# A fourth expert's slot products are moved ahead of the tile loop, and the weight loads are reordered for them

## The chip, the cores and the metric

The kernel runs on one core of one Trainium2 chip. The metric is the device time of one execution in microseconds (us), smaller is better. TensorE is called PE, VectorE DVE, ScalarE ACT, GpSimd POOL and SyncE SP. SP issues all the large loads, and POOL issues the indirect gathers and scatter-adds.

## What is computed

Attention over 8 heads with a local band and a few global columns, then two mixture-of-experts layers on the same 1536 tokens of width 512. The first is a soft one (every token is written as a mixture of 32 slots, four for each of 8 experts), the second sends each token to its two best experts.

```python
x = attention(q, k, v)                       # 1536 x 512
logits = x @ phi                             # 32 slots
slot_input = softmax(logits, axis=0).T @ x
slot_out[e] = relu(slot_input[e] @ w1[e]) @ w2[e]        # 8 experts, 4 slots each
x = softmax(logits, axis=1) @ slot_out       # layer 1's output: c @ slot_out

top2, weights = two best experts of noisy(x @ w_gate, x @ w_noise)
for e in range(8):                           # layer 2: tokens routed to expert e
    h = relu(x[mask] @ w1[e])                # 512 -> 1024
    out[mask] += weight * (h @ w2[e])        # 1024 -> 512
```

## The kernel before, in words

The first layer's output is never written out. Since x is c (1536 by 32) times the 32 slot rows s, the product x @ w1[e] of the second layer is c @ (s @ w1[e]). The 32-row product s @ w1[e] is called here the slot products of expert e. `slots_up(e)` makes them on PE (line 1509 of the kernel before, 16 matmuls, which the trace lists as 32) in PSUM bank 6, and `store_g(e)` on ACT copies them to `g_rows`. For e above 0, `slots_up(e)` waits until `store_g(e - 1)` is done, because there is one bank.

Tokens are sorted by expert into tiles of 128; here there are 28 tiles. For each tile POOL gathers 128 rows of c by an indirect DMA, ACT or POOL spreads them four times into `c4`, PE transposes them (`transpose_c4`, line 1261), DVE copies the result to `c4T`, PE forms the hidden values (`hidden`, line 1563), ACT applies relu and rounds (`hidden_high`, line 866), DVE keeps the remainder (`hidden_low`, line 1213), PE multiplies with w2 in split precision (`down`, lines 1574 and 1577, once for each half), ACT scales the sum (`store_y`, line 885) and POOL adds it to the output by an indirect DMA (line 705). The w2 weights of an expert must first be split: ACT writes the high part (`split_high`, line 733), DVE the low part (`split_low`, line 1127).

The weights of layer 2 pass through a ring of four buffers of 2 MB. Unit numbers are: `up1` and `down1` are the w1 and w2 of the second expert (expert 1), `up2` and `down2` of expert 2, `up3` and `down3` of expert 3, and so on. `up3` takes the buffer of `up1`, and can be loaded once the products of expert 1 are made. Units after the first few are loaded in two DMAs of 1 MB, of which the second is issued when the first has landed (`load_unit`, line 464); `down1` and `up2` are loaded in one DMA of 2 MB. SP issues the loads in the order of a written list (`order`, line 504), and waits for `c4_ready` (the first gather has arrived and been spread) before one of them.

Every engine has its program written by hand in one order, and waits on semaphores in that order. Before the tile loop PE makes the products of experts 0, 1 and 2, the routing tables, then for tile 0 the transpose and the hidden values, and then the transpose for tile 1. Inside the loop, `slots_up(e + 1)` stands ahead of the first tile's `down` of expert e for the later experts (`starts`, with `UP_EARLY` as the first such expert).

Of the kernel before, what the change touches and what calls it, by code (L numbers as in the profile page):

```python
# [16 lines left out]
def attention_two_moe_layers(nc, q, k, v, n_global, n_local, phi, a_w1, a_w2,  # L17
# [11 lines left out]
    E, _, F = a_w1.shape  # L29
# [18 lines left out]
    DC = DM // P  # L48
# [3 lines left out]
    FIRST = 4  # L52
    ROW = SLOTS + E
    ZEROED = 2 * 16
    UP_EARLY = 3
    DOWN_EARLY = 1
    AHEAD = 4
    REST = 4
# [2 lines left out]
    EARLY = 6  # L61
# [10 lines left out]
    with ExitStack() as ctx:  # L72
# [256 lines left out]
        g_ready, g_stored = sems("g_ready g_stored")  # L329
# [112 lines left out]
        def _(sp):  # L442
# [58 lines left out]


            down1, up2, down2, up3, down3, up4 = range(2 * E + RING2 - 1, 2 * E + RING2 + 5)
            order = [*range(EARLY, down1), up2, down1, up3, down2, *range(down3, 4 * E)]
            sums_before = {down3: 1, up4: 3}
            for n in order:
                m = before_unit(n)
                if n == EARLY + 2:

                    sp.wait_ge(heads_ready, UPB * B)  # L510
                if n == EARLY + DURING:

                    sp.wait_ge(part_ready, 1)
                if n == up3:

                    sp.wait_ge(c4_ready, 1)
                if n in sums_before:

                    sp.wait_ge(out_added, ZEROED + 16 * sums_before[n])
                if m is not None:  # L520

                    layer, which, e = units[m]
                    if (layer, which) == (1, 2):
                        sp.wait_ge(w_rest_stored, REST)
                        sp.wait_ge(w_lo_stored, FC * (e + 1) - REST)
                    else:
                        sp.wait_ge({(0, 1): hid_ready, (0, 2): soft_down_done, (1, 1): g_ready}[layer, which], e + 1)
                load_unit(n)
# [200 lines left out]
        def _(act):  # L729
# [42 lines left out]
            with nc.scalar.Else():  # L772
                for j in range(3):
                    store_qk(0, j, j, bank[FIRST_BANKS[j]])
                for u in range(UPB * B + 5):
                    p, i = divmod(u, QB)
                    if u < UPB * B:
                        off = P if i == 0 else 0
                        for h in range(2):
                            act.wait_ge(logits_ready, 2 * u + h + 1)  # L780
                            own = prob[u % 4][:, h, off:]
                            last = nc.scalar.activation(own, own, ACT.Exp, bias=neg_max[:, u % 2, h:h + 1], scale=-1.0,  # L782
                                                        accum_out=row_sum[:, u % 4, h:h + 1])
# [46 lines left out]
            def store_g(e):  # L830
                act.wait_ge(g_ready, e + 1)
                copy(g_rows[:, e, :], bank[6][:, 0:FR]).then_inc(g_stored, 1)
# [13 lines left out]
            for c in range(REST):  # L846
                split_low(c)
            store_g(1)

            def place_first(n):  # L850

# [18 lines left out]
            for half in range(2):  # L870
                hidden_high(half, 0, used=False)
            place_first(2)
            store_g(2)

            for n in range(FIRST):
                act.wait_ge(first_arrived[n], 16)
# [380 lines left out]
        def _(pe):  # L1257
# [21 lines left out]
            with pe.If(narrow == 0):  # L1279
                with pe.Fori(0, B) as b, pe.Fori(0, PAIRS // 2) as pp2:  # L1280
                    for s in range(2):
# [9 lines left out]
                        with pe.Fori(0, QB) as i:  # L1291
                            pe.wait_ge(all_q, UPB * b + 2 * QB * pp2 + i + (QB * s + 1))
                            for h in range(2):
                                n = 2 * UPB * b + 4 * QB * pp2 + 2 * i + (2 * QB * s + h + 1)
                                own = slice(h * HD, (h + 1) * HD)
                                for c in range(2):
                                    blocks = slice(c * QB // 2, (c + 1) * QB // 2)
                                    last = mm(bank[1 + c][:, 0:S // 2], q_block[own, :], kT[s][own, blocks, P:WIN],
                                              start=True, stop=True)
                                last.then_inc(all_scores, 1)  # L1300
                                pe.wait_ge(all_probs, n)
                                for c in range(QB):
                                    last = transpose(bank[4 + 2 * c // QB][:, (c % HALF) * P:(c % HALF + 1) * P],
                                                     prob_all[:, c * P:(c + 1) * P])
# [4 lines left out]
                                for c in range(QB):  # L1309
                                    last = mm(bank[6][own, 0:P], v_own[s][:, h, c, :], probT_all[:, c, :],  # L1310
                                              start=(c == 0), stop=(c == QB - 1))
                            last.then_inc(heads_ready, 1)
            with pe.Else():
# [53 lines left out]
                for u in range(UPB * B + 4):  # L1367
# [5 lines left out]
                    if 1 <= i <= 3 and p + 1 < NPAIR:  # L1373
                        n = 3 * (p + 1) + i - 1
# [25 lines left out]
            for c in range(DC):  # L1400
                for r in range(NG):
                    last = mm(bank[4][r * SLOTS:(r + 1) * SLOTS, 0:TG], phi_sb[:, c, :], xT[:, r * TPG:(r + 1) * TPG, c, :],
                              start=(c == 0), stop=(c == DC - 1))
# [7 lines left out]
            for t in range(TPG):  # L1411
                last = transpose(bank[5][:, t * P:(t + 1) * P], lT.rearrange("s (p t) -> s t p", t=TPG)[:, t, :])
# [9 lines left out]
            for t in range(TPG):  # L1422
                last = transpose(bank[6][:, t * P:(t + 1) * P], dT[:, t * P:(t + 1) * P])
# [6 lines left out]
            for t in range(TPG):  # L1430
                for r in range(NG):
                    last = mm(bank[0][r * SLOTS:(r + 1) * SLOTS, :], d_tok[:, (t * NG + r) * SLOTS:(t * NG + r + 1) * SLOTS],
                              x_sb[:, r * TPG + t, :], start=(t == 0), stop=(t == TPG - 1))
# [64 lines left out]
            last.then_inc(gate_log_ready, 1)  # L1498


            def slots_up(e):

                if e:

                    pe.wait_ge(g_stored, e)
                wait_unit(pe, (1, 1, e))
                for c in range(DC):
                    for r in range(NG):
                        last = mm(bank[6][r * SLOTS:(r + 1) * SLOTS, 0:FR], sT[:, c, :],  # L1509
                                  weights((1, 1, e))[:, c, r * FR:(r + 1) * FR], start=(c == 0), stop=(c == DC - 1))  # L1510
                last.then_inc(g_ready, 1)


            def split_rest(c):
# [31 lines left out]
            def transpose_c4(n, used=True):  # L1546
                pe.wait_ge(c4_ready, n + 1)
                if used:

                    pe.wait_ge(c4T_stored, n)  # L1550
                transpose(bank[7][:, 0:P], c4[:]).then_inc(c4T_ready, 1)
# [30 lines left out]
            pe.wait_ge(w_rest_stored, REST)  # L1582
            keep_warm(8)
            transpose_c4(0, used=False)
            pe.wait_ge(g_stored, 1)
            hidden(0, 0, used=False)
            transpose_c4(1)

            def period(i, e, first, last):
                up_ahead, _ = starts(e, first)  # L1590
# [48 lines left out]
```

## Time and profile before

| what | value |
|---|---|
| median of 3 runs (lowest, highest) | 393.13 us (390.88, 398.73) |
| the profiled execution's own time | 392.51 us |
| its span in the trace | 389.8 us |
| mean granted clock of PE | 0.971 of full |
| PE busy | 362.6 us, 93% |
| POOL, DVE, ACT busy | 213.3, 192.7, 170.4 us |

The span is what the trace covers; the execution's own time is 2.7 us longer. The attention takes the first third, layer 1 ends near 163 us, routing and tables last until about 187 us, and the 28 tiles fill the rest.

### The profile page before, as it was taken

How to read it: one execution, taken by the hardware profiler on the slowest of the kernel's cores; microseconds unless marked ns; L12 is line 12 of the kernel's file. 1: busy time of each engine (PE TensorE's matmuls, PEld its weight loads, DVE VectorE, ACT ScalarE, POOL GpSimd, SP SyncE). 2: the span in 40 equal slices, each digit the busy share in tenths (PEclk: the TensorE clock that was granted, in tenths of full speed). 3: DMA queues.
4: the chain of work that ended last, by engine and by line, in shares of the span. 5: the costliest groups of instructions: out<-in, count | busy, mean ns of one | idle time of the engine just before them, and what ended most of it. 6: DMA issues, size and time to landing. Idle time of an engine off the chain costs nothing.

```text
span 389.8 us, 8657 instructions
## 1 busy us (share of the span) xinstructions
PE 362.6 (93%) x2892; PEld 251.6 (65%) x2892; DVE 192.7 (49%) x639; ACT 170.4 (44%) x429; POOL 213.3 (55%) x422
## 2 busy tenths in 40 slices
PE   6899999999997999589799999999999999999990
PEld 5566666666564443256577777777777777777770
DVE  2699988888853011068172452623525426254210
ACT  2566777776541110043273453524525336253310
POOL 3568866667811040011446777747766576766741
PEclk9699999999999999889899999999999999999996
DMA  7987999999799999998577899876869762332432
GB/s 161 238 243 224 222 268 298 279 258 374 278 401 347 401 398 387 398 405 330 174 268 170 249 269 250 236 170 145 267 145 209 224 139 34 43 47 32 57 43 38
DMA packets 71976, 88.85 MB, mean 228 GB/s; under 512 B 41616, under 2 KB 42112, under 8 KB 71936
## 3 DMA queue, kind: packets, MB, share of 16 engines
q1 hardware_dynamic: 66448, 79.84, 62.7%
q0 software_dynamic: 5200, 8.49, 15.4%
q8 instruction: 23, 0.38, 0.4%
q14 instruction: 17, 0.14, 0.1%
q10 hardware_dynamic: 288, 0.00, 0.0%
HBM read 77.33 MB, written 10.99 MB: 227 GB/s over the span
## 4 chain that ended last, share of the span: by engine, by line
PE 59%; DVE 16%; issue 15%; DMA 8%; ACT 1%; DVEq 1%; POOL 0%; POOLq 0%; ACTq 0%
PE y_bank L1574 26%; PE y_bank L1577 13%; DMA weight_ring<-in_moe_w 6%; PE h_banks L1563 5%; DVE arena L1031 4%; DVE row_sum L1039 4%; PE bank L1509 3%; PE bank L1261 2%; PE y_bank L1478 2%; DVE row_inv L1053 2%; PE h_banks L1446 2%; PE h_banks L1261 1%; DVE arena L933 1%; DVE arena L1047 1%; DMA counts_i<-in_n_local 1%
## 5 line engine op out<-in xcount | busy, mean ns | idle before, releaser
L1213 DVE SCALAR_TENSOR_TENSOR hT_lo<-h_banks,hT_hi 128x512 fp32r<-128x512 f32 x56 | 38.5, 689 | 110.3 <-ACT hT_hi L866 104.8
L1574 PE MATMUL y_bank<-w_hi,hT_hi 128*128 128x512 f32 x224 | 91.6, 409 | 0.8 <-ACT hT_hi L866 0.8
L1574 PE MATMUL y_bank<-w_lo,hT_hi 128*128 128x512 f32 x224 | 88.2, 394 | 0.0
L866 ACT ACTIVATE hT_hi<-h_banks 128x512 fp32r<-128x512 f32 x56 | 33.4, 597 | 98.8 <-PE y_bank L1577 51.8
L610 POOL TENSOR_TENSOR arena<-arena,row_inv 128x512 f32<-128x512 f32 (+1 forms) x48 | 49.5, 1032 | 29.2 <-DVE row_inv L1053 27.1
L547 POOL TENSOR_TENSOR turn_mark<-turn_mark 128x1 f32<-128x1 f32 x135 | 41.4, 310 | 38.1 <-DMA out_rows<-arena,add_row 12.6
L1577 PE MATMUL y_bank<-w_hi,hT_lo 128*128 128x512 f32 x224 | 59.9, 389 | 0.0
L782 ACT ACTIVATE arena<-arena,neg_max 128x256 f32<-128x256 f32 (+1 forms) x96 | 46.3, 483 | 26.8 <-DVE neg_max L1031 25.8
L705 POOL DMA_INDIRECT out_rows<-arena,add_row x28 | 44.8, 1599 | 14.1 <-issue 13.0
L1574 PEld LDWEIGHTS y_bank<-w_hi,hT_hi 128*128 128x128 f32 x224 | 44.2, 197 | 11.2 <-issue 3.0
L1574 PEld LDWEIGHTS y_bank<-w_lo,hT_hi 128*128 128x128 f32 x224 | 42.8, 191 | 7.9
L1577 PEld LDWEIGHTS y_bank<-w_hi,hT_lo 128*128 128x128 f32 x224 | 42.1, 188 | 8.8
L1031 DVE CUSTOM_DVE_ANT_0 arena<-h_banks,arena 128x256 f32<-128x256 f32 (+1 forms) x96 | 34.4, 395 | 11.7 <-issue 11.4
L675 POOL DMA_INDIRECT c_fetched<-slot_rows,fetch_row x27 | 31.0, 1150 | 15.0 <-issue 14.9
L1127 DVE TENSOR_TENSOR w_lo<-weight_ring,w_hi 128x512 fp32r<-128x512 f32 x60 | 38.0, 692 | 0.0
L1330 PE MATMUL h_banks<-arena 64*128 64x256 f32 (+1 forms) x192 | 34.6, 425 | 1.8 <-DVE neg_max L1031 1.0
L733 ACT ACTIVATE w_hi<-weight_ring 128x512 fp32r<-128x512 f32 x64 | 34.8, 621 | 0.0
L1261 PE MATMUL y_bank<-ident,arena 128*128 128x128 f32 x190 | 32.2, 289 | 0.7 <-POOL arena L610 0.4
L1047 DVE COPY arena<-y_bank 128x512 f32<-128x512 f32 (+1 forms) x48 | 30.5, 635 | 1.5 <-PE y_bank L1261 1.5
L1261 PEld LDWEIGHTS y_bank<-ident,arena 128*128 128x128 f32 x190 | 20.1, 142 | 16.5 <-issue 11.1
L733 ACT ACTIVATE arena<-h_banks 128x512 f32<-128x512 f32 (+1 forms) x36 | 17.2, 496 | 15.8 <-PE h_banks L1261 8.2
L1330 PEld LDWEIGHTS h_banks<-arena 64*128 64x128 f32 x192 | 15.8, 191 | 10.7 <-issue 6.2
(196 smaller groups left out, 494.6 us busy)
## 6 DMA issues: line engine op xcount, KB each, us to landing
weight_ring<-in_moe_w SPq DMA_DIRECT2D x16, 2048.0 KB, 13.2
weight_ring<-in_moe_w SPq DMA_DIRECT2D x22, 1024.0 KB, 5.5
arena<-in_moe_w SPq DMA_DIRECT2D x5, 2048.0 KB, 12.1
arena<-in_q SPq DMA_DIRECT2D x16, 192.0 KB, 5.8
arena<-in_k SPq DMA_DIRECT2D x16, 192.0 KB, 5.4
arena<-in_v SPq DMA_DIRECT2D x8, 384.0 KB, 4.8
out_rows<-zero_row SPq DMA_DIRECT2D x2, 1536.0 KB, 10.4
out_rows<-arena,add_row POOLq DMA_INDIRECT x28
```

The lines of the kernel that those rows point to most:

```text
L547: g.tensor_tensor(turn_mark[:, turns[0]:turns[0] + 1], turn_mark[:, 0:1], turn_mark[:, 0:1], ALU.add)
L610: g.tensor_tensor(prob[u % 4][:, :, off:], prob[u % 4][:, :, off:], row_inv[:, u % 4, :].unsqueeze(2).to_broadcast([P, 2, WIN - off]), ALU ...
L705: pool.indirect_dma_start(out=out, out_offset=bass.IndirectOffsetOnAxis(ap=add_row[k][:, 0:1], axis=0), in_=y_sb[:, k], in_offset=None, bo ...
L733: return nc.scalar.activation(o, i, ACT.Copy)
L782: last = nc.scalar.activation(own, own, ACT.Exp, bias=neg_max[:, u % 2, h:h + 1], scale=-1.0, accum_out=row_sum[:, u % 4, h:h + 1])
L1031: vec.tensor_tensor_reduce(out=prob[u % 4][:, h, off:], in0=score_bank(u, h)[:, off:WIN], in1=bias8[:, 2 * pp + h, n0:n0 + nb], scale=-SCA ...
L1127: vec.tensor_tensor(w_lo[e % 2][:, c, :], weights((1, 2, e))[:, c, :], w_hi[e % 2][:, c, :], ALU.subtract).then_inc(w_lo_stored, 1)
L1213: vec.scalar_tensor_tensor(hidden_of(hT_lo, half), h_banks[half][:, :, 0:FR], 0.0, hidden_of(hT_hi, half), ALU.max, ALU.subtract).then_inc ...
L1261: return nc.tensor.transpose(o, i, ident[:])
L1330: last = mm(score_bank(u, h)[:, off:WIN], qT[s][own, i * P:(i + 1) * P], kT[s][own, i, off:], start=True, stop=True)
L1574: mm(y_of(i), hT_hi[:, n, :], w[e % 2][:, n, :], start=(n == 0 and w is w_hi), stop=False)
L1577: last = mm(y_of(i), hT_lo[:, n, :], w_hi[e % 2][:, n, :], start=False, stop=(n == FC - 1))
```

## The change

The slot products of expert 3 leave the tile loop. Their 16 matmuls are issued before it, in two halves: eight after the transpose for tile 0, and eight after the transpose for tile 1. ACT stores the products of expert 2 earlier (they must be out of the bank) and those of expert 3 where it stored those of expert 2. SP loads `up3` ahead of `down1`, and the wait for the first gather moves from `up3` to `down1`.

```diff
-    UP_EARLY = 3
+    UP_EARLY = 4
...
-            order = [*range(EARLY, down1), up2, down1, up3, down2, *range(down3, 4 * E)]
+            order = [*range(EARLY, down1), up2, up3, down1, down2, *range(down3, 4 * E)]
...
-                if n == up3:
+                if n == down1:
 
                     sp.wait_ge(c4_ready, 1)
...
             store_g(1)
+            store_g(2)
...
             place_first(2)
-            store_g(2)
+            store_g(3)
...
-            def slots_up(e):
-
-                if e:
+            def slots_up(e, chunks=range(DC)):
+
+                if e and 0 in chunks:
 
                     pe.wait_ge(g_stored, e)
                 wait_unit(pe, (1, 1, e))
-                for c in range(DC):
+                for c in chunks:
                     for r in range(NG):
                         last = mm(bank[6][r * SLOTS:(r + 1) * SLOTS, 0:FR], sT[:, c, :],
                                   weights((1, 1, e))[:, c, r * FR:(r + 1) * FR], start=(c == 0), stop=(c == DC - 1))
-                last.then_inc(g_ready, 1)
+                if DC - 1 in chunks:
+                    last.then_inc(g_ready, 1)
...
             transpose_c4(0, used=False)
+            slots_up(3, range(DC // 2))
             pe.wait_ge(g_stored, 1)
             hidden(0, 0, used=False)
             transpose_c4(1)
+            slots_up(3, range(DC // 2, DC))
```

PE before the tile loop, from the products of expert 2 to the first `down`, in the program before (bank is PSUM bank 6 for the products and bank 7 for the transposes, c holds the spread rows):

```order
L1509 MATMUL bank<-weight_ring,arena 32x256 x16
L1266 MATMUL h_banks<-ident 128x128 x8
L1261 MATMUL bank<-ident,c 128x128
L1563 MATMUL h_banks<-c4T,arena 128x128 x8
L1261 MATMUL bank<-ident,c 128x128
L1574 MATMUL y_bank<-w_hi_53,hT_hi 128x512
```

The same place in the changed program:

```order
L1510 MATMUL bank<-weight_ring,arena 32x256 x16
L1267 MATMUL h_banks<-ident 128x128 x8
L1262 MATMUL bank<-ident,c 128x128
L1510 MATMUL bank<-weight_ring,arena 32x256 x8
L1565 MATMUL h_banks<-c4T,arena 128x128 x8
L1262 MATMUL bank<-ident,c 128x128
L1510 MATMUL bank<-weight_ring,arena 32x256 x8
L1576 MATMUL y_bank<-w_hi_53,hT_hi 128x512
```

Eight matmuls of the products now stand ahead of the hidden values of tile 0, and eight ahead of its `down`.

SP's loads around the change, in the program before (in_moe2_w1 are up units, in_moe2_w2 down units; the first row is `up2`):

```order
L464 DMA weight_ring<-in_moe2_w1 128x4x1024 [waits g_ready]
L464 DMA weight_ring<-in_moe2_w2 128x8x512 [waits soft_down_done]
L464 DMA weight_ring<-in_moe2_w1 128x2x1024 [waits g_ready,c4_ready]
L464 DMA weight_ring<-in_moe2_w1 128x2x1024 [waits unit_loaded2]
L464 DMA weight_ring<-in_moe2_w2 128x4x512 [waits w_lo_stored,w_rest_stored]
```

And in the changed program:

```order
L464 DMA weight_ring<-in_moe2_w1 128x4x1024 [waits g_ready]
L464 DMA weight_ring<-in_moe2_w1 128x2x1024 [waits g_ready]
L464 DMA weight_ring<-in_moe2_w1 128x2x1024 [waits unit_loaded2]
L464 DMA weight_ring<-in_moe2_w2 128x8x512 [waits soft_down_done,c4_ready]
L464 DMA weight_ring<-in_moe2_w2 128x4x512 [waits w_lo_stored,w_rest_stored]
```

The two halves of `up3` now wait for no gather, and the 2 MB of `down1` do.

## Rows read from the trace of the kernel before

**Rows 1.** The page: busy time of PE, share of the span, instructions.

```profile
PE 362.6 (93%) x2892; PEld 251.6 (65%) x2892; DVE 192.7 (49%) x639; ACT 170.4 (44%) x429; POOL 213.3 (55%) x422
```

**Rows 2.** Chain of waits, tile loop: start us, us, what.

```profile
229.74 1.81 PE y_bank L1574 x8
...
232.46 0.66 PE h_banks L1563 x16
233.11 0.26 PE bank L1261
...
236.12 1.86 PE bank L1509 x32
237.99 2.04 PE y_bank L1574 x8
```

**Rows 3.** Timeline of PE: start us, us, instructions, idle time before and its releaser.

```profile
176.14 1.93 PE L1509 MATMUL bank<-weight_ring,arena 128*32 128x256 f32 x32
...
187.13 0.33 PE L1261 MATMUL bank<-ident,c 128*128 128x128 f32 x1 [0.86 <-ACT c L733]
189.73 0.77 PE L1574 MATMUL y_bank<-w_hi,hT_hi 128*128 128x512 f32 x1 [0.81 <-ACT hT_hi L866]
...
194.05 0.73 PE L1563 MATMUL h_banks<-c4T,arena 32*128 32x128 f32 x16
```

**Rows 4.** Windows: stretch, length, busy time of five engines, PEclk, DMA share, GB/s.

```profile
188.00:190.00 2.00, 1.19 (x18) 0.91 (x19) 0.39 (x1) 1.28 (x3) 1.40 (x3) 0.82 0.80 258
190.00:192.00 2.00, 2.00 (x6) 1.54 (x6) 1.10 (x3) 0.07 (x1) 1.05 (x1) 0.50 0.78 290
192.00:194.00 2.00, 2.00 (x8) 1.42 (x6) 0.00 (x0) 0.71 (x3) 0.00 (x0) 0.82 0.58 93
```

**Rows 5.** Timeline of SP's issues; an x2 row covers two, from the first's start.

```profile
187.10 0.37 SPq L464 DMA_DIRECT2D weight_ring<-in_moe_w  x1
...
191.87 0.89 SPq L464 DMA_DIRECT2D weight_ring<-in_moe_w  x2
...
199.94 0.37 SPq L464 DMA_DIRECT2D weight_ring<-in_moe_w  x1
```

**Rows 6.** Timeline of POOL: gathers of tiles 0, 2 and 3.

```profile
183.62 1.67 POOL L664 DMA_INDIRECT arena<-slot_rows,fetch_i  x1 [8.09 <-DVE fetch_i L1195]
...
186.93 1.01 POOL L664 DMA_INDIRECT arena<-slot_rows,fetch_i  x1 [0.30 <-issue]
188.25 1.01 POOL L664 DMA_INDIRECT arena<-slot_rows,fetch_i  x1 [0.30 <-issue]
```

**Rows 7.** Timeline of ACT: spreads of tiles 0 and 2, first splits of down1.

```profile
186.77 0.31 ACT L733 ACTIVATE c<-arena 128x128 f32<-128x128 f32 x1 [5.41 <-DMA arena<-slot_rows,fetch_i]
...
192.08 0.31 ACT L733 ACTIVATE c<-arena 128x128 f32<-128x128 f32 x1 [2.00 <-DMA arena<-slot_rows,fetch_i]
...
194.94 0.60 ACT L866 ACTIVATE hT_hi<-h_banks 128x512 fp32r<-128x512 f32 x1 [2.16 <-PE h_banks L1563]
195.44 2.19 ACT L733 ACTIVATE w_hi<-weight_ring 128x512 fp32r<-128x512 f32 x4
```

**Rows 8.** DMA queues (packets, MB, share) from 178.5 to 180.5 us.

```profile
q0 software_dynamic: 80, 0.25, 33.0%
```

**Rows 9.** The same from 188 to 190.9 us.

```profile
q1 hardware_dynamic: 221, 0.91, 87.5%
```

**Rows 10.** The same from 190.9 to 192.4 us.

```profile
q0 software_dynamic: 95, 0.06, 22.9%
```

**Rows 11.** Timeline of DVE, second remainder of tile 1.

```profile
198.85 0.68 DVE L1213 SCALAR_TENSOR_TENSOR hT_lo<-h_banks,hT_hi 128x512 fp32r<-128x512 f32 x1
```

**Rows 12.** Timelines of PE (hidden values of tile 2) and POOL (scatter-adds).

```profile
200.45 0.73 PE L1563 MATMUL h_banks<-c4T,arena 32*128 32x128 f32 x16
...
353.04 1.60 POOL L705 DMA_INDIRECT out_rows<-arena,add_row  x1 [0.28 <-issue]
...
382.15 1.56 POOL L705 DMA_INDIRECT out_rows<-arena,add_row  x1 [0.54 <-issue]
```

## The prediction

> **What bounds the kernel now.** I read the page first: PE is busy for 93% of the span [rows 1]. Then the chain of waits: from 200 us to 374 us every piece of it is PE, one tile after another, with no wait between them, so a PE instruction that leaves this stretch is worth its full length. The slot products of expert 3 stand in it at 236.12 us for 1.86 us, and the `down` half behind them takes 2.04 us where it otherwise takes 1.81 us [rows 2]. They cost the loop 1.86 + 0.23 = **2.09 us**.
>
> Then the stretch just before the loop, on PE's own timeline. Here PE is not full: it idles 0.86 us until the first gather is spread and 0.81 us for the first rounded hidden values [rows 3]. The change puts the two halves of the products into these holes. The granted clock shows that the holes have an after-effect: it is 0.82, 0.50 and 0.82 in the three stretches of 2 us from 188 us [rows 4]. With 0.50 as the lower level of 1.2 GHz, that is 0.72 + 2.0 + 0.72 = 3.4 us at half clock, roughly 189.3 to 192.7 us.
>
> Last, SP's and POOL's timelines with the DMA queues, since the new work needs 2 MB that were not there at this time before.
>
> **Part 1, the loop.** Removed: one `slots_up` and one `store_g`. Gain 2.09 us on the path. What could keep it from the end is the chain of scatter-adds, which closes the kernel. Between the scatter at 353.04 us and the last at 382.15 us there are five steps of 5.82 us on average [rows 12], against 200.45 - 194.05 = 6.40 us for a tile on PE [rows 3, 12]. So the scatters catch up with PE between two slots of products, and a gain on PE reaches the end whole.
>
> **Part 2, when `up3` lands.** Its buffer is free when the products of expert 1 are made, 176.14 + 1.93 = 178.1 us [rows 3]. SP has nothing else before it. SP issues right after the semaphore it waits for: 187.10 us, with the spread done at 187.08 us [rows 5, 7]. So the first half is issued at 178.15 us. A half takes 191.87 - 187.10 = 4.77 us from issue to landing [rows 5], and in this stretch it shares the engines with the write of the gathered table, 0.25 MB [rows 8], which at the 400 GB/s of a full stretch is 0.6 us. First half down at 183.5 us, second at **188.3 us**. The trace bounds this: without sharing 187.7 us, and with the 8.07 us that the next two halves took (191.87 to 199.94) in place of 4.77 + 4.77 us, 186.8 us at the earliest.
>
> PE would reach the first half of the products at 187.4 us in any case, so `up3` alone holds it for about 0.9 us.
>
> **Part 3, the first gather.** Before, no load ran between the last weights of `down1` and the gather, and `c4_ready` guarded this. The gather issued at 183.62 us was there at 186.77 us, 3.15 us later; the gather issued at 186.93 us, beside the first half of `up3`, was there only at 192.08 us, 5.15 us later [rows 6, 7]. The queues show why: from 188 to 190.9 us queue 1 moved 221 packets and queue 0, the gathers' own, none; queue 0 has its 95 packets from 190.9 us on, as the half runs out [rows 9, 10]. Now the second half of `up3`, issued at 183.5 us, lies over the first gather in the same way. Bounds for its arrival: 186.77 us (no harm) and 183.62 + 5.15 = 188.8 us. I take **188.7 us**, since the gather at 186.93 us is the near case: same size, same kind of load. The spread ends at 189.0 us, and PE transposes at 189.05 us instead of 187.13 us.
>
> The Trainium skill, in "DMA: Bandwidth & Descriptors" (Queues, rings and completion order), says that each DMA engine takes turns between queues but drains a whole packet, typically 9 to 17 descriptors and at most 64, before it turns. A 1 MB half is 16 rows of 4 KB for each engine, one packet by that rule, and the trace agrees: the gather waited for one half. By the rule the gather is held as long as the half lasts, which speaks against this change.
>
> **Part 4, PE up to the first `down`.** At full clock the work from the transpose is 0.26 (transpose) + 0.93 (half of 1.86) + 0.66 (hidden) + 0.26 + 0.93 = 3.04 us [rows 2]. Before, the stretch at half clock followed the idle time from 186 us on; that idle time is longer now, so I keep the stretch where it is. From 189.05 us there is 0.24 us of work until 189.3 us, 1.7 us of work in the 3.4 us of half clock, and the other 1.1 us after it: `down` starts at 193.8 us instead of 189.73 us [rows 3]. Now it runs at full clock. A tile's 6.40 us less 0.66 and 0.26 leave 2.74 us for each half of `down`, so it ends at **196.55 us**, against 194.1 us before, where the next hidden values start [rows 3]. So the loop starts **2.4 us** later, not 4.1 us, because the slow stretch falls on the moved work instead of on `down`. ACT isn't late: the hidden values end near 192.5 us, their rounding 0.75 us later.
>
> **Part 5, `down1`.** It was issued straight behind `up2`, before the gathers, and is now issued after `c4_ready`, 189.0 us. The nearest price for 2 MB at this place is the 8.07 us from 191.87 to 199.94 us [rows 5], so it lands near 197.1 us. ACT asks for it after rounding tile 1's first half, at 195.44 us before [rows 7] and 197.9 us now. The cover is 0.8 us thin; if it fails, what is late next is the second rounding of tile 1, which stands behind the splits on ACT, and then tile 2's hidden values on PE. From the start of the splits to the end of that remainder it takes 199.53 - 195.44 = 4.1 us [rows 7, 11], and PE wants it at 200.45 + 2.4 = 202.9 us [rows 12]. So `down1` may land as late as 198.7 us before PE notices. Cost here: nothing. `down2` and what follows keep their order; the first of them is issued near 189.4 us instead of 192.4 us, so no later need suffers.
>
> `store_g(2)` on ACT is 0.4 us in a wait of 5.41 us [rows 7] and costs nothing; `store_g(3)` falls in the wait for the loop's first hidden values.
>
> **The sum.** -2.09 + 2.4 = +0.3 us: 392.8 us for the profiled execution of 392.51 us. That execution lies 0.6 us under the median of the runs shown, so in terms of the median 393.4 us.
>
> **The rivals.**
>
> *The load hardly harms the gather.* Then `c4_ready` stays at 187.1 us, and `up3` at 188.3 us is the later one. PE starts the 2.78 us of work behind the transpose there: 1.0 us until 189.3 us, 1.7 us at half clock until 192.7 us, `down` from 192.8 us, its end 195.5 us. Loop later by 1.4 us, net -0.7 us. If besides the denser work kept the clock up, `down` would start at 191.1 us and end at 193.85 us, net -2.3 us. For it: the gathers are 20 KB each. Against: the empty queue 0 in [rows 9]. Time 390.8 to 392.4 us in the median's terms. Chance 0.22.
>
> *ACT stands behind `down1`, or behind the fourth gather.* ACT waits for all four gathers before tile 1's rounding. The fourth, issued at 188.25 us [rows 6], now meets `down1` and the first half of `down2` behind it. If `down1` lands at 201 us, which is 12 us after its issue and not the 8.07 us of the near row, PE loses 201 - 198.7 = 2.3 us, and with the clock dropping in the hole another 1.7 us (3.4 us at half clock, as in [rows 4]). Net +2.6 to +4.3 us, slower: 396 to 397.7 us. The point from which it decides is a landing of `down1`, or of the fourth gather, past 198.7 us or 197.8 us. For it: a margin of 1.6 us on a guess of 8 us. Against: only 2 MB are in the way, with nothing ahead of them. Chance 0.23.
>
> By the typical packet of the Trainium skill ("DMA: Bandwidth & Descriptors", same section) the fourth gather would be served after 9 to 17 of `down1`'s 64 rows for each engine, near 191 us; by the row above, only when the load is through, near 197 us. Neither alone reaches the point.
>
> *The clock.* The longer idle time (186.3 to 189.0 us) may bring a second slow stretch, or the slow stretch may start later and fall on `down` again. This adds 1.7 us to the forecast: +2.0 us. Chance 0.1, counted within the forecast's range.
>
> **Chances and range.** The forecast (-0.5 to +2 us) has 0.55, the two rivals 0.22 and 0.23. About 2% (7.8 us) is what a measurement of this kernel can tell from no change, and the three runs before alone spread over that. No case reaches it by itself: faster by over 2% 0.02, within 0.92, slower 0.06, for a stall with clock loss larger than I priced or a disturbed median. The range runs from the fast rival with its clock kept, 390.0 us, to the slow rival's far end, 397.8 us.
>
> **What would show it.** In the changed profile: (1) SP issues a half of `up3` near 178.2 us and the next near 183.5 us; (2) ACT's first spread starts near 188.7 us, released by the gather, not 186.8 us; (3) the first eight product matmuls, 16 in the trace, follow the transpose at about 189.3 us, at half clock; (4) the first `down` starts at about 193.8 us and hidden values of tile 1 at 196.5 us; (5) the splits of `down1` on ACT start near 198 us, with PE unbroken after them; (6) no products between two `down` halves in the first tile of expert 2, near 238.6 us. It is wrong if (2) stays at 186.8 us, if PE idles after 197 us, or if the slow stretch moves. Then the sum changes by 1 to 4 us, which the profile shows better than the runs.

## The result, and the profile after

| | before | changed |
|---|---|---|
| first job, median (lowest to highest) | 392.76 us (390.88 to 398.73), n = 4 | 397.5 us (393.21 to 399.25), n = 4 |
| ratio | | 1.0101, 95% interval 1.0059 to 1.0143 |
| second job, median (lowest to highest) | 392.45 us (388.9 to 400.75), n = 29 | 399.94 us (396.79 to 401.91), n = 6 |
| ratio | | 1.0124, interval 1.0046 to 1.0202 |

By the two ratios the change costs 4 to 5 us, 1%: less than the 2% of "no change", clear of noise, and slower. The second job's medians lie further apart, 7.5 us; with six executions of the changed kernel its interval reaches from 0.5% to 2.0%. The range held the first median, 0.3 us from its upper end; the second job's lies above it. The ratios compare fast executions with fast ones and leave the disturbed ones out. The profile of the first job is of its slowest execution (399.25 us, span 397.5 us) and is read for the stretch before the loop. The main readings of the loop rest on the second job's profile (396.79 us, span 394.2 us); that is its fastest execution of six, so it need not show all of the loss.

First SP's issues in the changed kernel, as [rows 5] had them before:

```profile
178.34 0.37 SPq L464 DMA_DIRECT2D weight_ring<-in_moe_w  x1
...
183.58 0.37 SPq L464 DMA_DIRECT2D weight_ring<-in_moe_w  x1
...
188.99 0.99 SPq L464 DMA_DIRECT2D weight_ring<-in_moe_w  x2
```

The halves of `up3` are issued at 178.34 and 183.58 us, `down1` at 188.99 us, all within 0.2 us of the prediction. The queues from 183.6 to 186.5 us:

```profile
q1 hardware_dynamic: 131, 0.54, 65.4%
```

There is no packet of queue 0, though the first gather was issued at 183.82 us. Before, it was the same after 188 us [rows 9]. PE's timeline, against [rows 3]:

```profile
189.01 0.33 PE L1262 MATMUL bank<-ident,c 128*128 128x128 f32 x1 [2.54 <-ACT c L733]
189.27 1.79 PE L1510 MATMUL bank<-weight_ring,arena 128*32 128x256 f32 x16
190.99 1.24 PE L1565 MATMUL h_banks<-c4T,arena 32*128 32x128 f32 x16
...
192.57 1.20 PE L1510 MATMUL bank<-weight_ring,arena 128*32 128x256 f32 x16
...
196.64 0.73 PE L1565 MATMUL h_banks<-c4T,arena 32*128 32x128 f32 x16
```

The first half of the products runs mostly at half clock (1.79 us; the same matmuls take 1.07 us at full clock in the kernel with half of `up3` ahead), the hidden values of tile 1 start at 196.64 us (predicted 196.55). Up to here the sum was right. ACT and then POOL:

```profile
188.65 0.31 ACT L733 ACTIVATE c<-arena 128x128 f32<-128x128 f32 x1 [3.71 <-DMA arena<-slot_rows,fetch_i]
...
199.08 2.20 ACT L733 ACTIVATE w_hi<-weight_ring 128x512 fp32r<-128x512 f32 x4 [0.94 <-DMA weight_ring<-in_moe_w]
...
201.66 0.30 ACT L733 ACTIVATE c<-arena 128x128 f32<-128x128 f32 x1
```

```profile
202.04 0.25 POOL L547 TENSOR_TENSOR turn_mark<-turn_mark 128x1 f32<-128x1 f32 x1 [10.54 <-ACT c L733]
```

`down1` landed at 199.0 us, 10 us after its issue. The spread of tile 3 stands behind four of its splits on ACT, and POOL's loop waits for that spread: it starts at 202.04 us, against 198.78 us before. Of these 3.3 us, PE's own later start makes 2.6 us (196.64 against 194.05 us), since ACT's rounding ahead of the splits waits for PE. In the second job's profile ACT doesn't wait for `down1` at all (its splits start at 197.40 us, right behind the rounding), and POOL's loop starts at 200.72 us. That is 4.71 us behind tile 1's hidden values on PE, against 4.73 us before: POOL starts no later with respect to PE than it did.

In the loop, PE no longer runs unbroken. Its waits (us in total, times, longest) from 175 us to the end, in the first job's profile:

```profile
PE bank L1262 <- POOL c L717: 4.3, 3, 3.6
PE bank L1262 <- ACT c L733: 2.5, 1, 2.5
```

The second of these rows is the first gather, before the loop. The second job's profile shows where, on PE's timeline:

```profile
249.90 0.47 PE L1262 MATMUL bank<-ident,c 128*128 128x128 f32 x1 [2.08 <-POOL c L717]
258.58 0.33 PE L1262 MATMUL bank<-ident,c 128*128 128x128 f32 x1 [0.66 <-POOL c L717]
```

and what POOL waited for:

```profile
237.10 0.19 POOL L547 TENSOR_TENSOR turn_mark<-turn_mark 128x1 f32<-128x1 f32 x1 [2.14 <-DMA out_rows<-arena,add_row]
246.42 0.23 POOL L547 TENSOR_TENSOR turn_mark<-turn_mark 128x1 f32<-128x1 f32 x1 [3.61 <-DMA out_rows<-arena,add_row]
255.59 0.19 POOL L547 TENSOR_TENSOR turn_mark<-turn_mark 128x1 f32<-128x1 f32 x1 [2.88 <-DMA out_rows<-arena,add_row]
```

PE waits for the spread of a tile's rows, POOL makes that only after its scatter-add, and the scatter-add waits until the one before has landed. The queues show why a landing is late. The scatter-add issued at 237.87 us (1.60 us long) stood still while queue 1 carried weights; these are the queues from 239 to 243 us, where queue 0 has no packet, and from 243.5 to 246 us:

```profile
q1 hardware_dynamic: 532, 1.40, 99.6%
```

```profile
q0 software_dynamic: 163, 0.26, 55.7%
q1 hardware_dynamic: 68, 0.21, 23.3%
```

The windows (stretch, length, busy time of PE, PEld, DVE, ACT, POOL, granted clock, DMA share, GB/s) show the clock behind the wait:

```profile
245.00:250.00 5.00, 2.92 (x27) 2.11 (x26) 4.09 (x7) 3.40 (x7) 2.97 (x6) 0.98 0.69 217
250.00:255.00 5.00, 5.00 (x16) 4.02 (x17) 0.29 (x1) 0.37 (x1) 1.92 (x6) 0.68 0.94 276
```

**The books**, from this profile. I cut at three marks: the products of expert 2 on PE (181.13 us; before 182.35), tile 1's hidden values (196.01; before 194.05) and PE's last four matmuls (383.10; before 378.82).

| piece | before | changed | difference | made of |
|---|---|---|---|---|
| up to the first mark | 182.35 | 181.13 | -1.22 | the attention, not touched |
| to tile 1's hidden values | 11.70 | 14.88 | +3.18 | late gather, moved products |
| the loop | 184.77 | 187.09 | +2.32 | -2.09 products, +2.74 waits for POOL, +1.7 clock |
| the tail | 10.98 | 11.10 | +0.12 | |
| span | 389.8 | 394.2 | +4.4 | |

The clock's 1.7 us are half of the 3.4 us at half clock behind the first wait, which 0.98 and 0.68 in the windows make (5 x 0.02 x 2 + 5 x 0.32 x 2 = 3.4). The first job's profile, of the slowest execution, gives +0.20, +2.39 (14.09 us), +5.08 (189.85 us) and +0.03, together +7.7 us; there the waits are 4.3 us.

### The profile page after: what moved, and what is told of

Same layout as the page of the kernel before. It is cut to its first block, busy times and chain, and to the rows that moved or that the text cites. A ratio compares the mean times of both kernels' runs of the same rounds, so it can differ in the third digit from the quotient of the medians.

```text
span 397.5 us, 8657 instructions
## 1 busy us (share of the span) xinstructions
PE 365.4 (92%) x2892; PEld 253.1 (64%) x2892; DVE 193.0 (49%) x639; ACT 170.7 (43%) x429; POOL 212.8 (54%) x422
## 4 chain that ended last, share of the span: by engine, by line
PE 39%; issue 24%; DVE 17%; POOL 10%; DMA 7%; POOLq 1%; ACT 1%; DVEq 1%; ACTq 0%
PE y_bank L1576 15%; PE y_bank L1579 8%; DMA weight_ring<-in_moe_w 6%; DVE arena L1032 4%; DVE row_sum L1040 4%; POOL c_fetched L675 3%; PE h_banks L1565 3%; POOL turn_mark L547 2%; PE bank L1510 2%; POOL out_rows L705 2%; PE y_bank L1479 2%; DVE row_inv L1054 2%; PE h_banks L1447 2%; PE bank L1262 1%; PE h_banks L1262 1%
## 5 line engine op out<-in xcount | busy, mean ns | idle before, releaser
L547 POOL TENSOR_TENSOR turn_mark<-turn_mark 128x1 f32<-128x1 f32 x135 | 42.3, 316 | 45.7 <-DMA out_rows<-arena,add_row 20.0
L1579 PE MATMUL y_bank<-w_hi,hT_lo 128*128 128x512 f32 x224 | 60.7, 393 | 0.0
L1032 DVE CUSTOM_DVE_ANT_0 arena<-h_banks,arena 128x256 f32<-128x256 f32 (+1 forms) x96 | 34.5, 395 | 11.7 <-issue 11.4
```

The lines of the kernel that those rows point to most:

```text
L547: g.tensor_tensor(turn_mark[:, turns[0]:turns[0] + 1], turn_mark[:, 0:1], turn_mark[:, 0:1], ALU.add)
L1032: vec.tensor_tensor_reduce(out=prob[u % 4][:, h, off:], in0=score_bank(u, h)[:, off:WIN], in1=bias8[:, 2 * pp + h, n0:n0 + nb], scale=-SCA ...
L1579: last = mm(y_of(i), hT_lo[:, n, :], w_hi[e % 2][:, n, :], start=False, stop=(n == FC - 1))
```

## The experiments

Theory P (in later forms P2 and P3) puts the loss on POOL: it has no slack once PE stops pausing for expert 3's products. Theory S puts all of it on the later start of PE's loop and a chance clock drop. Each ratio is to the kernel before in the same job, with its 95% interval. In tables and text, "start" is the second piece above (before 11.70 us) and "loop" the third (before 184.77 us), of the run's profile.

**The changed kernel again** (no edit).

> The changed kernel as it is, timed beside the others. Theory P (POOL has no slack left between 235 and 270 us once PE no longer pauses there for expert 3's products, and PE waits for POOL's spread rows): +3 to +5 us against before, PE waits of 2 us or more for POOL's spread between 235 and 270 us, not the same in every run. Theory S (the whole loss is the later start of the loop, 2.5 us, plus a clock that drops by chance): +0.5 us in a profile without a clock drop, and no PE wait for POOL.

Measured: 1.0124 (1.0046 to 1.0202); its profile is read above. It has a wait for POOL of 2.08 us, as theory P said and S did not. Theory P had no term for the clock drop behind it.

**The loads alone.**

```diff
-            order = [*range(EARLY, down1), up2, down1, up3, down2, *range(down3, 4 * E)]
+            order = [*range(EARLY, down1), up2, up3, down1, down2, *range(down3, 4 * E)]
-                if n == up3:
+                if n == down1:
```

> The kernel before with the new order of loads alone (the fourth expert's up weights ahead of the second expert's down weights, the gather's guard moved), products where they were. Both theories: the first gather is spread at 188.7 us instead of 186.8 us, so PE's first transpose is 1.9 us later and the first down matmul near 191.6 us. Theory S: +1.9 to +2.5 us on the whole. Theory P: the same +1.9 to +2.5 us, because the pause for the products is still at 236 us and PE never waits for POOL's spread; if POOL waits show up here too, the load order and not the missing pause is their cause.

Measured: 396.63 us median, ratio 1.0101 (1.0058 to 1.0144). Start 12.88 us. PE, with the products still in the loop:

```profile
254.86 0.47 PE L1261 MATMUL bank<-ident,c 128*128 128x128 f32 x1 [3.02 <-POOL c L717]
```

The ratio is 4.0 us (2.3 to 5.6 us), above the 1.9 to 2.5 us that both theories expected. In this profile the wait for POOL is there with the pause in place, and PE waits 0.94 us for the second rounding of tile 1 besides. But the profile is of an execution of 402.92 us, 6 us above the median, so these waits are not shown for the typical one. By the ratios the order of the loads alone costs about what the whole change costs. That by itself does not show the gain in the loop lost: the moved products also lengthen the start (14.88 against 12.88 us), by about what they should save in the loop. What the new order adds beyond the later start stays open here; the next run and the last pair test the gain itself.

**The pause put back** into the changed kernel.

```diff
+                if first and e == 2:
+                    pe.wait_ge(g_stored, 4)
+                    for _ in range(8):
+                        mm(bank[6][:, 0:P], ident[:], ident[:], start=True, stop=True)
```

> The changed kernel with 8 idle matmuls (128x128 fp32 of the identity, 16 in the trace, some 2 us) into the products' bank where the loop made expert 3's products before; they compute nothing. Theory P: no slower than the changed kernel, within 0.5 us, since PE would have waited there for POOL anyway; the PE waits for POOL's spread between 235 and 270 us shrink by 2 us or vanish. Theory S: 2 us slower than the changed kernel.

Measured: 1.0125 (1.0079 to 1.0171), against 1.0124 without the idle matmuls; the medians are 396.37 and 399.94 us. The ratios alone could hide 2 us, the medians speak against a loss. In the profiles the loop is 184.93 us, as long as the kernel before's (184.77 us) and 2.2 us shorter than without the pause, and POOL's loop again starts 4.72 us behind tile 1's hidden values. PE's wait for POOL is down to

```profile
PE bank L1262 <- POOL c L717: 0.4, 1, 0.4
```

from 2.7 us, and there is no clock drop in the loop. So some 2 us of PE time at this place cost nothing in the changed kernel. Theory S, which wanted 2 us more than the changed kernel, does not fit this.

**An earlier start of POOL's loop,** in the changed kernel and in the one before: ACT spreads tile 3's rows before the splits.

```diff
                     hidden_high(0, i + 1)
+                if first and e == 0:
+                    place_first(FIRST - 1)
                 if down_ahead:
...
                     hidden_high(1, i + 1)
-                if first and e == 0:
-                    place_first(FIRST - 1)
```

> The changed kernel with the spread of tile 3's rows on ACT moved ahead of the second expert's first four weight splits, so that POOL's loop starts at about 198.3 us instead of 202.0 us. Theory P: POOL has 3.5 us more lead, the PE waits for its spread vanish, and the time falls by 2.5 to 4.5 us to within 1 us of the kernel before. Theory S: no change (within 0.5 us).

Measured: 1.0054 (1.0002 to 1.0105), median 395.1 us; the changed kernel is at 1.0124 in the same job, and the two intervals overlap. In the profile POOL's loop starts 3.0 us earlier (197.71 against 200.72 us), the wait for POOL shrinks from 2.7 to 1.4 us, with no clock drop, and the loop is 184.20 us. The direction is P's. By the ratios the fall is 2.7 us, at the lower end of what I expected, and the kernel stays 2.1 us above the one before, where I expected 1 us: a start 3.0 us earlier took away only half of the wait.

> The kernel before with the spread of tile 3's rows on ACT moved ahead of the second expert's first four weight splits, so POOL's loop starts near 196.5 us instead of 198.8 us. Theory P2 (revised: POOL's chain of scatter-adds and spreads between 235 and 270 us sets the pace together with PE, so what counts is when POOL's loop starts; a late start of it is paid in full, and PE time saved in the loop is not): no change against before in the profile's kind of execution, since PE never waited for POOL there, at most 1 us faster in the median through executions in which it did. Theory S (only the start of PE counts): exactly no change.

Measured: 0.9988 (0.9952 to 1.0023). POOL's loop starts at 196.52 us, but PE's loop takes 184.75 us, as before. An earlier start of POOL is worth something only where it is missing.

**Only half of `up3` ahead of the gather.** SP waits for `c4_ready` between the halves and not before `down1`; PE's first half of the products waits for the first half of the weights (the lines for these two are left out below), its second half stands behind the first half of tile 0's `down`.

```diff
                         sp.wait_ge(unit_loaded[slot_of(n)], loaded(n) - 16)
+                        if units[n] == (1, 1, 3):
+                            sp.wait_ge(c4_ready, 1)
...
             transpose_c4(1)
-            slots_up(3, range(DC // 2, DC))
...
                 down(0, i, e)
+                if first and e == 0:
+                    slots_up(3, range(DC // 2, DC))
```

> The changed kernel with only the first half of the fourth expert's up weights ahead of the first gather, the second half behind the guard, and the second half of the products after the first half of the first down. The gather is spread near 186.9 us again and the first transpose is at 187.2 us. PE's loop: tile 1's hidden values near 195.4 us (before 194.05, changed kernel 196.6). Theory S: 195.4 - 194.05 - 2.1 = 0.7 us faster than before. Theory P2: POOL's loop starts near 199.5 us, 0.7 to 1.5 us later than before, and the products' time in the loop brings nothing, so 0 to +1.5 us against before; in either case 1.5 to 3 us better than the changed kernel.

Measured: 1.0124 (1.0059 to 1.0188). PE and ACT:

```profile
193.97 0.73 PE L1568 MATMUL h_banks<-c4T,arena 32*128 32x128 f32 x16
...
203.04 0.82 PE L1568 MATMUL h_banks<-c4T,arena 32*128 32x128 f32 x16 [2.62 <-DVE hT_lo L1213]
```

```profile
199.04 2.19 ACT L732 ACTIVATE w_hi<-weight_ring 128x512 fp32r<-128x512 f32 x4 [2.96 <-DMA weight_ring<-in_moe_w]
```

The gather is early again and tile 1's hidden values are at 193.97 us, but `down1` is behind half of `up3` in the queue. ACT stands 2.96 us at its splits, with the second rounding of tile 1 behind them, and PE waits for it: the slow rival of the prediction, at its place and 0.3 us past its point of 198.7 us. My expectation had no term for it.

The same with the earlier spread:

> The kernel of e5 with the spread of tile 3's rows moved ahead of the splits as well. POOL's loop starts near 197.5 us. Theory P2: the lead of POOL covers part of the missing pause, so this is the best of the kernels with the products ahead, 0.7 us faster than before to 0.5 us slower. Theory S: same time as e5.

Measured: 1.013 (1.009 to 1.017). PE's wait for the rounding is 2.9 us here, and the earlier spread does nothing against it. Both theories missed this.

**The late `down1` alone:** the old order, but the guard moved from `up3` to `down1`.

```diff
-                if n == up3:
+                if n == down1:
```

> The kernel before with one edit: the wait for the first gather stands before the second expert's down weights instead of the fourth expert's up weights, in the old order. The first gather is as early as before; the down weights are issued at 187.1 us instead of 171.1 us and land near 194.5 to 196 us. It separates the late down weights from the late gather. If the late gather is the cause: no change against before (within 0.5 us). If the late down weights and the later start of POOL's loop behind their splits are: +1 to +3 us, and PE waits for POOL's spread appear.

Measured: 1.0224 (1.018 to 1.0268), median 399.89 us, the largest ratio of all. The first gather is early (the first transpose waits 0.86 us, as before), so the late first gather is not needed for a loss of this size; issuing `down1` late is enough, and costs more than I expected. Its profile has PE waits,

```profile
PE bank L1261 <- POOL c L717: 2.5, 3, 1.5
PE bank L1261 <- ACT c L733: 1.6, 2, 0.9
PE h_banks L1563 <- DVE hT_lo L1213: 1.4, 1, 1.4
```

but is of its fastest execution (394.41 us, the others 399.6 to 403.2 us), so it doesn't show all of the loss. Its start is 10.00 us, 1.70 us shorter than before, since the clock did not drop there, and its loop 189.92 us, 5.15 us longer.

**The spread ahead of the scatter-add** on POOL, in both kernels: the block that waits for `c4T_ready` and `c_arrived` and writes `c4` moves up, ahead of

```diff
+                [the spread of the gathered rows into slot_gate and c4]
                 pool.wait_ge(out_added, 16 * i + ZEROED)
                 pool.wait_ge(y_stored, i + 2)
                 turn()
                 pool.indirect_dma_start(...)
-                [the spread of the gathered rows into slot_gate and c4]
```

> The kernel before with one reordering in POOL's program for a tile: the spread of the gathered rows, on which PE's transpose waits, stands ahead of the scatter-add (which waits until the scatter-add of the tile before has landed) instead of behind it. Theory P2: in the kernel before PE never waited for POOL in the profile, so no change there, 0 to 1.5 us faster in the median through the executions in which it did. If POOL's chain of scatter-adds itself (not the order in it) sets the pace, slower by up to 3 us, since each scatter-add now starts later.

Measured: 1.0055 (1.0011 to 1.0098), slower and within what the second case of the expectation allowed. In its profile PE waits 3.1 us for ACT's rounding in the loop, which it never did in the loop before.

> The changed kernel with the same reordering. Theory P2 (PE stalls because its next tile's spread is queued on POOL behind a scatter-add that waits for a landing delayed by weight loads): the PE waits for POOL's spread between 235 and 270 us vanish, so do the clock drops behind them, and the loop from tile 1's hidden values to the end is 2 us shorter than before's 195.75 us: against before +2.4 - 2.1 = +0.3 us (the sum of the prediction), 3 to 5 us faster than the changed kernel. If the scatter-adds' own chain is the limit: no better than the changed kernel, and PE or ACT waits for the output buffers appear instead.

Measured: 1.013 (1.0075 to 1.0185). ACT's waits in the changed kernel with this edit:

```profile
ACT arena L885 <- DMA out_rows<-arena,add_row: 33.2, 8, 8.8
```

and PE's:

```profile
PE y_bank L1575 <- ACT hT_hi L866: 4.1, 3, 3.2
PE bank L1261 <- POOL c L708: 1.3, 3, 0.5
```

Theory P2's forecast falls, and the second case came. The wait for the spread is down to 1.3 us and another has its place: ACT can't store a tile's sum until an output buffer is free, that is until a scatter-add has landed (this wait is 0.6 us in the changed kernel). Not the order in POOL's program is the limit, but the chain of scatter-adds itself. The profile is of an execution of 400.73 us, near the median of 399.55 us.

**Fewer bytes beside the scatter-adds.**

```diff
+                    cols = slice(0, to.shape[2] // 16) if h and n >= 2 * E + RING2 + 3 else slice(None)
-                    sp.dma_start(to[:, own], of[:, own]).then_inc(unit_loaded[slot_of(n)], 16)
+                    sp.dma_start(to[:, own, cols], of[:, own, cols]).then_inc(unit_loaded[slot_of(n)], 16)
```

> The changed kernel, but of the second half of every weight unit from the fourth expert's down weights on only a sixteenth of the columns is loaded (the rest of those weights is left out, so 1 MB of each 2 MB stays away from the DMA engines). Theory P3 (the chain of scatter-adds, each of which waits for the landing of the one before, paces the loop between 235 and 275 us because weight loads hold up their landings): the PE waits for POOL vanish and the time falls to the predicted sum, 5 us below the changed kernel, within 1 us of the kernel of e10b. Rival: the scatter-adds are slow by themselves (POOL's instructions), not through the loads: the waits stay and so does the time.

> The kernel before with the same weights left out, as the base of e9b. Theory P3: no change to 1 us faster than before, since PE had no waits for POOL there in the profiled execution. The difference e9b - e10b is then +0.3 us (range -0.5 to +1.5 us), against the +4 to +5 us of the changed kernel over before. Rival: e9b - e10b stays near +4 us.

Measured: the changed kernel 1.0034 (1.0005 to 1.0062), median 393.3 us; the one before 0.9999 (0.9967 to 1.0031), 391.71 us. The gap between the two falls from 1.0 to 1.2% to 0.35% (1.0034 over 0.9999), which is 1.4 us. POOL's waits for a landing from 200 to 300 us, in the changed kernel and in this one, are

```profile
POOL turn_mark L547 <- DMA out_rows<-arena,add_row: 13.0, 7, 3.6
```

```profile
POOL turn_mark L548 <- DMA out_rows<-arena,add_row: 4.7, 4, 1.8
```

From 235 to 275 us the windows of the two are

```profile
235.00:275.00 40.00, 37.26 (x248) 28.44 (x245) 13.53 (x26) 15.16 (x27) 22.48 (x57) 0.96 0.69 194
```

```profile
235.00:275.00 40.00, 40.00 (x278) 30.73 (x277) 16.47 (x31) 17.79 (x32) 29.64 (x69) 1.00 0.65 140
```

PE is full, at full clock. The loop takes 182.89 us against 184.74 us in the kernel before with the same loads: 1.85 us of the 2.09 us of the products are earned here. So theory P3 holds for the loop: with the full loads the gain is lost, with light ones it is kept, and what shrank in between is POOL's waits for scatter-adds to land. The edit takes bytes from everything that moves after `down3`, so the landings are not the only thing it changed, but in the loops of these profiles PE waits for nothing but POOL with the full loads (2.74 us), and for 0.17 us in all with the light ones. The spread between executions goes too: the kernel before with light loads ran from 390.47 to 393.66 us in 12 executions, beside it the kernel before from 389.58 to 400.37 us in 23. The profiles put the remaining difference at 0.2 us (start 13.96 against 11.93 us, loop 1.85 us less), the runs at 1.4 us; this last 1 us is open.

## Why the prediction was right, and where it was wrong

A result within 2% of no change came, as the prediction put at 0.92. That the range held the first median is luck. The forecast of +0.3 us missed by about 4 us, and the range reached that far only because of a rival whose mechanism did not occur. Its upper end also rests on a slip: the slow rival's +4.3 us is a difference to the kernel before, and was added to the forecast (393.4 us) instead of to the median before (393.1 us). Added rightly it ends at 397.4 us, just under the measured 397.5 us. The step that failed is in part 1, "a gain on PE reaches the end whole".

- **`up3` and the first gather** (parts 2 and 3): right. Issues within 0.2 us; the spread started at 188.65 us (predicted 188.7).
- **The fourth gather** came between the two prices. ACT's copy of the gates waits for all four:

```profile
194.83 0.23 ACT L733 ACTIVATE arena<-arena 128x32 f32<-128x32 f32 x1 [0.60 <-DMA arena<-slot_rows,fetch_i]
```

 It was issued at 188.46 us and was there at 194.8 us, before `down1` (199.0 us) and after the 191 us that the prediction estimated from the typical packet of the Trainium skill ("DMA: Bandwidth & Descriptors", Queues, rings and completion order). The trace agrees with the rule in that a large load is not finished first, and not with its typical size.
- **PE up to the loop** (part 4): right to 0.1 us in the first profile. In the second it is 0.8 us more, since PE waited 3.30 us for the first gather and not 2.54 us. The slow stretch itself is not a fixed cost: in the profiles of the late `down1` and of the spread first in the kernel before, where PE has the old program, the clock stayed full and the start was 10.0 us instead of 11.7 us. The prediction took the stretch as given.
- **`down1`** (part 5): mis-sized. I took 8.07 us from issue to landing, it was 10.0 us. The first half of `down2` is issued 0.6 us behind it, and gathers are in the way too. PE did not wait for it, as part 5 said. Part 5 left out one consumer, the spread of tile 3, which stands on ACT behind four splits and starts POOL's loop. In the first profile ACT's wait for `down1` (0.94 us) moved it by about 0.7 us beyond PE's own delay, in the second by nothing. So in the changed kernel the late `down1` is not shown to be the cause; the kernel with only this edit shows that it can cost much.
- **The loop** (part 1): this step failed, and the 2.09 us came back as 2.74 us of waits and 1.7 us of clock. "A gain on PE reaches the end whole" rested on scatter-adds from 353 us on, 5.82 us apart, where no weights are loaded. Before, between 202.45 and 264.25 us, ten scatter-adds are 6.87 us apart on average, PE's tiles there (6.40 us, and the products once in nine) 6.63 us. Two of the starts are

```profile
248.87 1.60 POOL L705 DMA_INDIRECT out_rows<-arena,add_row  x1 [0.27 <-issue]
258.46 1.60 POOL L705 DMA_INDIRECT out_rows<-arena,add_row  x1 [0.58 <-issue]
```

 9.6 us apart. In this stretch POOL's chain and PE pace the loop together, and the 1.86 us that PE spends on expert 3's products are time in which POOL catches up. The profiles with the same distance between POOL's start and PE's show it: with the pause the loop is 184.8 us (before) and 184.9 us (pause put back), without it 187.1 us and not 182.7 us. With light loads the pause can go: 182.9 us.
- **The forecast** of +0.3 us was some 4 us short. The terms missing are 2.7 us of waits for POOL and 1.7 us of clock behind them (4.3 us of waits in the slowest execution). The 2.09 us are in the books, and are spent again at once.
- **The rivals.** The fast one did not come. The slow one has its price right (+2.6 to +4.3 us) but not its place: PE was never held by the second rounding in the two profiles of the changed kernel. It was in the two kernels with half of `up3` ahead of the gather (2.62 and 2.94 us), and for less in those with the loads alone (0.94 us), with the late `down1` (1.38 us) and with the spread first in the changed kernel (0.33 us). What decides the real mechanism is how far POOL's chain can fall behind before PE notices, and the prediction had no term for it.

What stays open is how the loss splits between the late gather, the late `down1` and the missing pause. The order of the loads alone cost 4 us, of which a later start explains 1.2 us in its one profile; the rest is not profiled in a typical execution. The late `down1` alone gave more than both together (1.0224 against 1.0101 for the loads alone), so the two don't add. That it matters how the loads and the scatter-adds fall on each other is my reading; no run separates it. No version here beats the kernel before; the earlier spread in it (0.9988) equals it.

## What to carry to other kernels

An engine without waits in the trace can still be paced by two things at once. Before pricing PE time saved in a loop, compare the step of every other chain in the same stretch, with the transfers that run there, and find how far it may fall behind before the busy engine waits. A pause of one engine can be what lets the other catch up. When a load is moved, list every instruction that stands behind its first consumer on that engine, and who starts on those.

## What the runs showed of the hardware

- A small indirect transfer beside a 1 MB load was served when the load ran out, for gathers (5.15 us against 3.15 us) as for the scatter-add issued at 237.87 us: queue 0 had no packet from 239 to 243 us, and 163 from 243.5 to 246 us.
- With half of the bytes of the late loads left out, the times of the kernel before spread over 390.47 to 393.66 us instead of 389.58 to 400.37 us. That the scatter-adds carry this spread is likely and not shown.
- A wait of PE of 2.08 us in the loop was followed by 3.4 us at half clock (0.68 over the 5 us from 250 us), which cost 1.7 us more than the wait; waits of 0.40 us (with the pause put back) and 1.01 us (with the earlier spread) by none. But the length of a wait does not decide it alone. In the changed kernel with the spread first, a wait of 3.17 us left the clock full:

```profile
261.96 0.49 PE L1575 MATMUL y_bank<-w_hi,hT_hi 128*128 128x512 f32 x1 [3.17 <-ACT hT_hi L866]
```

```profile
255.00:260.00 5.00, 3.30 (x21) 2.25 (x15) 0.00 (x0) 0.00 (x0) 0.64 (x4) 1.00 0.95 288
260.00:265.00 5.00, 3.04 (x16) 2.28 (x16) 1.49 (x3) 1.66 (x3) 3.40 (x6) 1.00 0.56 203
```
